# Two attention steps per turn of TensorE's loop, with another order of loads, casts and first steps

## The reference

```python
def _attn_ref(q, k, v, s):                       # (2, 8, 576, 64), s: (2, 8, 576)
    scores = scale * np.matmul(q, k.transpose(0, 1, 3, 2))
    s_pos = np.maximum(s, 0.0)
    cum = np.cumsum(s_pos, axis=-1)
    bias = -(cum[:, :, :, None] - cum[:, :, None, :])
    scores = np.where(causal, -1000000000.0, scores + np.minimum(bias, 0.0))
    attn = softmax of scores over the last axis
    return np.matmul(attn, v)

def reference(**kwargs):
    x = attention output, reshaped to (1152, 512)
    x = _moe_ref(x, ...)     # 8 experts, top 2 of noisy logits; relu(x @ w1[e]) @ w2[e]
    return _moe2_ref(x, ...) # 8 experts, dense, weights from 8 Sinkhorn steps
```

## Time and profile before

| | us |
|---|---|
| median of 3 runs | 1208.1 |
| lowest, highest | 1206.51, 1209.63 |
| profiled execution: its own time | 1210.0 |
| profiled execution: span of the core | 1208.3 |
| PE busy | 1191.1 (99%) |
| DVE busy | 696.7 (58%) |
| ACT busy | 421.9 (35%) |
| POOL busy | 259.8 (22%) |

### The profile page before, as it was taken

How to read it: one execution, slowest core, us unless ns; L and a number is a source line. 1 busy time by engine, 2 the same in 40 slices (tenths; PEclk the granted TensorE clock), 3 DMA queues, 4 the chain that set the end, 5 groups by cost and what they waited for, 6 DMA issues and landing times.

```text
span 1208.3 us, 20170 instructions
## 1 busy us (share of the span) xinstructions
PE 1191.1 (99%) x7149; PEld 1059.8 (88%) x7149; DVE 696.7 (58%) x1579; ACT 421.9 (35%) x887; POOL 259.8 (22%) x307
## 2 busy tenths in 40 slices
PE   8999899999999989999999999999999999999998
PEld 5888798888888888989889899899898898898997
DVE  5554676544544451566575575575575665755753
ACT  5666344433444341233133232242241231332320
POOL 8777111111101357111011011010010010110110
PEclk9999899999999999999999999999999999999999
DMA  7770644444545420012120210211211201202102
GB/s 171 164 186 21 246 136 156 153 153 180 179 171 201 160 79 1 1 36 79 62 70 0 69 55 15 69 35 35 69 35 35 69 14 56 69 0 69 35 0 78
DMA packets 40326, 103.04 MB, mean 85 GB/s; under 512 B 4814, under 2 KB 23758, under 8 KB 38106
## 3 DMA queue, kind: packets, MB, share of 16 engines
q1 hardware_dynamic: 33850, 85.97, 22.9%
q0 software_dynamic: 3360, 11.01, 3.1%
q10 hardware_dynamic: 3072, 5.51, 1.3%
HBM read 87.74 MB, written 10.30 MB: 81 GB/s over the span
## 4 chain that ended last, share of the span: by engine, by line
PE 94%; DVE 2%; POOL 1%; DMA 1%; ACT 1%; issue 0%; POOLq 0%; DVEq 0%
PE bank L1132 10%; PE bank L1131 10%; PE bank L1130 9%; PE bank L1086 9%; PE bank L1084 9%; PE bank L1085 9%; PE bank L909 5%; PE bank L911 5%; PE bank L910 5%; PE bank L891 5%; PE bank L893 4%; PE bank L892 4%; PE bank L820 4%; PE bank L803 1%; PE bank L769 1%; PE bank L804 1%
## 5 line engine op out<-in xcount | busy, mean ns | idle before, releaser
L740 POOL TENSOR_TENSOR part2l<-raw_part,part2h 128x512 fp32r<-128x512 f32 x56 | 72.5, 1294 | 589.7 <-ACT part2h L1365 589.7
L1132 PE MATMUL bank<-part2h,partl 128*128 128x512 f32 x504 | 198.6, 394 | 0.0
L1131 PE MATMUL bank<-part2l,parth 128*128 128x512 f32 x504 | 197.6, 392 | 0.0
L1130 PE MATMUL bank<-part2h,parth 128*128 128x512 f32 x504 | 195.6, 388 | 0.0
L1820 DVE SCALAR_TENSOR_TENSOR x_sb<-bank,share_now,x_sb 128x512 f32<-128x512 f32 x126 | 94.4, 750 | 159.4 <-PE bank L1132 159.4
L1086 PE MATMUL bank<-x_forms,forml 128*128 128x288 f32 x448 | 132.1, 295 | 0.0
L1084 PE MATMUL bank<-x_forms,formh 128*128 128x288 f32 x448 | 131.9, 294 | 0.0
L1085 PE MATMUL bank<-x_forms,formh 128*128 128x288 f32 x448 | 131.8, 294 | 0.0
L1505 DVE SCALAR_TENSOR_TENSOR hl<-bank,hh 128x336 fp32r<-128x336 f32 (+1 forms) x88 | 45.8, 521 | 131.4 <-ACT hh L1242 123.8
L891 PE MATMUL bank<-xTh,w1h 128*128 128x336 f32 (+1 forms) x352 | 115.8, 329 | 0.7 <-DVE xTl L1485 0.5
L892 PE MATMUL bank<-xTl,w1h 128*128 128x336 f32 (+1 forms) x352 | 113.8, 323 | 0.0
(11 more groups left out here) (229 smaller groups left out, 2455.3 us busy)
## 6 DMA issues: line engine op xcount, KB each, us to landing
raw<-in_w SPq DMA_DIRECT2D x15, 2048.0 KB, 9.2
raw_part<-in_w1b SPq DMA_DIRECT2D x14, 1024.0 KB, 6.0
raw_part<-in_w2b SPq DMA_DIRECT2D x14, 1024.0 KB, 6.1
k_raw<-in_kT SPq DMA_DIRECT2D x16, 288.0 KB, 5.3
y_dram<-x_sb ACTq DMA_DIRECT2D x16, 256.0 KB
q_raw<-in_qT SPq DMA_DIRECT2D x8, 288.0 KB, 5.1
q_two<-w2l SPq DMA_DIRECT2D x8, 288.0 KB, 6.0
x_dram<-x_sb SPq DMA_DIRECT2D x1, 2304.0 KB, 10.0
```

Source lines behind the costliest of these rows:

```text
L1130: pe.matmul(dst, parth[:, l, ts], part2h[:, l, :], start=(l == 0), stop=False)
L1131: pe.matmul(dst, parth[:, l, ts], part2l[:, l, :], start=False, stop=False)
L1132: mm = pe.matmul(dst, partl[:, l, ts], part2h[:, l, :], start=False, stop=(l == FL - 1))
```

## The change

The four jobs and what they compute stay as they are. What changes is order and place:

- **PE's loop** goes over pairs of steps from k = 0 on: both `rough`, both sets of turns, both `scores`, both `mix`, both token turns. The other engines keep their single steps.
- **The first steps** are laid out anew (`FILL` = 10, `roughs_at`, `turns_at`): the loop starts at k = -10, 7 instead of 10 `rough` stand before the first `scores`, and the distance of 13 steps is reached at k = 6. PE and DVE both follow `roughs_at`.
- **`HIGH_AHEAD`** goes from 19 to 21: ACT rounds k and q of heads 2 to 7 (and the first expert's w1) two steps earlier. The q of head 1 is rounded at k = -7 and -6.
- **Loads** of head 1 on are issued as k, k, q. `load_raw(1)` now stands behind the four `first_cum`, and `double_k(1)` behind the store of the sums, the load of v and `load_cum(1)`.
- **The running sums' low part** is computed before the rounding of k for the first head; that rounding (64x1152) moves from DVE to ACT.
- **Constant rows** of ring place 1 move from POOL to DVE (three memsets), and those of ring place 2 come earlier on POOL.
- `WARM_UPS` goes from 8 to 6 and `WARM_TOP2` from 18 to 15. Two semaphores are merged into one.

The numbers of the lines in the changed kernel are higher: `rough` L786, `turn_max` L800, `scores` L820 and L821, `mix` L837, `keep_warm` L843; on ACT `high_k` L1195, `high_q` L1204, `place_max` L1187, the exponentials L1176 to L1179.

The diff:

```diff
         MAX_BANKS, MAX_AT, SCORES_AT, OUT_AT = 3, 3, 4, 6
-        ROUGH_AHEAD, SCORES_AHEAD = 13, 4
-
-        WARM_UPS = 8
-        WARM_TOP2, WARM_RANKS, WARM_GATHER, WARM_BACK = 18, 4, 6, 29
+        ROUGH_AHEAD, SCORES_AHEAD, FILL = 13, 4, 10
+
+        WARM_UPS = 6
+        WARM_TOP2, WARM_RANKS, WARM_GATHER, WARM_BACK = 15, 4, 6, 29
...
-        HIGH_AHEAD, LOW_AHEAD = 19, 14
+        HIGH_AHEAD, LOW_AHEAD = 21, 14
...
         def high_at(k):
 
+            if k in (-7, -6):
+                return (1, 1, k + 7)
             h, part = divmod(k + HIGH_AHEAD, HEAD)
...
+        def roughs_at(k):
+
+            lags = {0: (10,), 1: (11, 12), 2: (13,), 3: (14, 15), 4: (16,), 5: (17, 18)}
+            r = lags[k] if k in lags else (k + FILL,) if k < 0 else (k + ROUGH_AHEAD,)
+            return [i for i in r if i < ALL]
+
         def turns_at(k):
 
+            early = {-7: (0, 0), -5: (0, 1), -2: (1, 0), 0: (1, 1)}
             first, rest = divmod(k + ROUGH_AHEAD - 4, STEPS), divmod(k + ROUGH_AHEAD - 7, STEPS)
-            found = []
-            if first[1] == 0 and 0 <= first[0] < G:
+            found = [early[k]] if k in early else []
+            if first[1] == 0 and 2 <= first[0] < G:
                 found.append((first[0], 0))
-            if rest[1] == 0 and 0 <= rest[0] < G:
+            if rest[1] == 0 and 2 <= rest[0] < G:
                 found.append((rest[0], 1))
...
             def load_raw(h):
                 w = h % RAW_RING
                 sp.dma_start(k_raw[0:HD, w, :], kT[h]).then_inc(k_loaded[w], 16)
-                sp.dma_start(q_raw[:, w, :], qT[h]).then_inc(q_loaded[w], 16)
+                if h == 0:
+                    sp.dma_start(q_raw[:, w, :], qT[h]).then_inc(q_loaded[w], 16)
                 sp.dma_start(k_raw[HD:P, w, :], kT[h]).then_inc(k_again[w], 16)
+                if h:
+                    sp.dma_start(q_raw[:, w, :], qT[h]).then_inc(q_loaded[w], 16)
...
             load_raw(0)
-            load_raw(1)
             sp.wait_ge(aug_ready, 2)
             sp.wait_ge(cum_high, 1)
             first_cum(HD, cum_h, 0, cum_first)
...
             first_cum(HD + 1, cum_l, 1, cum_loaded[0])
+            load_raw(1)
             double_q(0)
...
+            load_v(0)
+            load_cum(1)
             double_k(1)
-            load_cum(1)
-            load_v(0)
             sp.wait_ge(low, LOWS)
             load_raw(2)
...
+            for i, w in enumerate((0, 2)):
                 pool.memset(k_top[w][HD:P, :].bitcast(F32), 1.0).then_inc(aug_ready, 1)
                 pool.memset(q_top[w][HD:P, :].bitcast(F32), 0.0).then_inc(q_rows_clear, 1)
-                pool.wait_ge(q_rows_clear, w + 1)
-                pool.memset(q_top[w][HD:HD + 2, :].bitcast(F32), 1.0).then_inc(q_rows_ready, 1)
-
-            constant_rows(0)
-            constant_rows(1)
...
-            for k in range(-ROUGH_AHEAD, ALL):
...
-                if k + ROUGH_AHEAD < ALL:
-                    rough(k + ROUGH_AHEAD)
...
+            for ks in [(k,) for k in range(-FILL, 0)] + [(k, k + 1) for k in range(0, ALL, 2)]:
+                for k in ks:
+                    for r_ in roughs_at(k):
+                        rough(r_)
+                    if k < -SCORES_AHEAD:
+                        keep_warm(BANK // 2)
+                for k in ks:
+                    for n, part in turns_at(k):
+                        turn_max(n, part)
+                for k in ks:
+                    if 0 <= k + SCORES_AHEAD < ALL:
+                        scores(k + SCORES_AHEAD)
+                for k in ks:
+                    if k >= 0:
+                        mix(k)
+                for k in ks:
+                    if k >= EARLY_AT:
+                        if k == EARLY_AT:
+                            pe.wait_ge(head_done, G - 1)
+                        turn_token(SP_, k - EARLY_AT, x_sb)
...
             act.copy(cum_h[0:G, :], cum_s[0:G, :]).then_inc(cum_high, 1)
+            act.wait_ge(k_loaded[0], 16)
+            act.copy(k_top[0][0:HD, :], k_raw[0:HD, 0, :]).then_inc(k_first, 1)
+            for half in range(B):
+                high_q(0, half)
             for h in range(2):
                 for half in range(B):
-                    high_q(h, half)
-                for half in range(B):
                     high_k(h, half)
...
-            v.wait_ge(k_loaded[0], 16)
-            v.tensor_copy(k_top[0][0:HD, :], k_raw[0:HD, 0, :]).then_inc(k_first, 1)
             v.wait_ge(cum_high, 1)
             v.tensor_tensor(cum_l[0:G, :], cum_s[0:G, :], cum_h[0:G, :].bitcast(F32), ALU.subtract).then_inc(cum_low, 1)
+            v.memset(k_top[1][HD:P, :].bitcast(F32), 1.0).then_inc(k_rows_ready, 1)
+            link(v.memset(q_top[1][HD:P, :].bitcast(F32), 0.0))
+            v.memset(q_top[1][HD:HD + 2, :].bitcast(F32), 1.0).then_inc(q_second_ready, 1)
...
-                if k + ROUGH_AHEAD < ALL:
-                    row_max(k + ROUGH_AHEAD)
+                for r_ in roughs_at(k):
+                    row_max(r_)
```

More of the change, by code:

```diff
@@ L202, in build @@
         q_rows_ready = sem("q_rows_ready")
+        k_rows_ready = sem("k_rows_ready")
+        q_second_ready = sem("q_second_ready")
         k_again = [sem(f"k_again{w}") for w in range(RAW_RING)]
@@ L227, in build @@
         first_w1 = [sem(f"first_w1_{c}") for c in range(DC - 1)]
-        gates_loaded = sem("gates_loaded")
-        noise_loaded = sem("noise_loaded")
+        gates_noise_loaded = sem("gates_noise_loaded")
         dve = sem("dve")
@@ L439, in load_cum @@
                 w = h % HEADS_RING
-                if h < HEADS_RING:
-                    sp.wait_ge(aug_ready, 2 + h)
                 if h == 1:
+                    sp.wait_ge(k_rows_ready, 1)
                     sp.wait_ge(cum_stored, 32)
+                if h == 2:
+                    sp.wait_ge(aug_ready, 3)
                 sp.dma_start(k_top[w][HD:HD + 2, :].rearrange("r (b s) -> r b s", b=B).bitcast(F32),
@@ L587, in _, with q_ones @@
             pool.wait_ge(const_ready, 6)
-            def constant_rows(w):
+            def q_ones(w):
+                pool.memset(q_top[w][HD:HD + 2, :].bitcast(F32), 1.0).then_inc(q_rows_ready, 1)
+            for i, w in enumerate((0, 2)):
                 pool.memset(k_top[w][HD:P, :].bitcast(F32), 1.0).then_inc(aug_ready, 1)
                 pool.memset(q_top[w][HD:P, :].bitcast(F32), 0.0).then_inc(q_rows_clear, 1)
-                pool.wait_ge(q_rows_clear, w + 1)
-                pool.memset(q_top[w][HD:HD + 2, :].bitcast(F32), 1.0).then_inc(q_rows_ready, 1)
-            constant_rows(0)
-            constant_rows(1)
-            pool.wait_ge(aug_ready, HEADS_RING)
-            pool.wait_ge(q_rows_ready, 2)
+                pool.wait_ge(q_rows_clear, i + 1)
+                if w == 0:
+                    q_ones(0)
+            pool.wait_ge(aug_ready, 3)
+            pool.wait_ge(q_rows_ready, 1)
             def low_part(h, c, k):
@@ L641, in _ @@
                     pool.wait_ge(low, LOWS)
-                    constant_rows(2)
-                    pool.wait_ge(q_rows_ready, 3)
+                    q_ones(2)
+                    pool.wait_ge(q_rows_ready, 2)
                 if k >= 0:
@@ L754, in rough @@
                         pe.wait_ge(k_doubled[w], 16 * (h // HEADS_RING + (w > 0)))
-                    if h < HEADS_RING:
-                        pe.wait_ge(q_rows_ready, h + 1)
+                    if h == 1:
+                        pe.wait_ge(q_second_ready, 1)
+                    elif h < HEADS_RING:
+                        pe.wait_ge(q_rows_ready, 1 if h == 0 else 2)
                     if h == 0:
@@ L958, in _ @@
                 keep_warm(BANK)
-            for k in range(-ROUGH_AHEAD, ALL):
-                if k + ROUGH_AHEAD < ALL:
-                    rough(k + ROUGH_AHEAD)
-                if k < -SCORES_AHEAD:
-                    keep_warm(BANK // 2)
-                for n, part in turns_at(k):
-                    turn_max(n, part)
-                if 0 <= k + SCORES_AHEAD < ALL:
-                    scores(k + SCORES_AHEAD)
-                if k >= 0:
-                    mix(k)
-                if k >= EARLY_AT:
-                    if k == EARLY_AT:
-                        pe.wait_ge(head_done, G - 1)
-                    turn_token(SP_, k - EARLY_AT, x_sb)
+            for ks in [(k,) for k in range(-FILL, 0)] + [(k, k + 1) for k in range(0, ALL, 2)]:
[18 more added lines that the diff above has]
+                        turn_token(SP_, k - EARLY_AT, x_sb)
             pe.sem_inc(xg_turned, SLOTS_T)
@@ L1196, in _ @@
             act.copy(cum_h[0:G, :], cum_s[0:G, :]).then_inc(cum_high, 1)
+            act.wait_ge(k_loaded[0], 16)
+            act.copy(k_top[0][0:HD, :], k_raw[0:HD, 0, :]).then_inc(k_first, 1)
+            for half in range(B):
+                high_q(0, half)
             for h in range(2):
                 for half in range(B):
-                    high_q(h, half)
-                for half in range(B):
```

(6 more changed lines are left out.)

6 lines of the change are left out of this document (3 added, 3 removed).

## The result

The changed kernel is slower: 1252.6 us median of four runs (1246.49 to 1256.81) against 1207.6 before on the same chip, a ratio of 1.0365 with a 95% interval of 1.0342 to 1.0388. The forecast was 1209.4, the range 1204.5 to 1212.8. Where runs of one kernel lie far apart, a ratio counts only those near its fastest, so the runs are given beside it. The profiled execution took 1246.49.

The account below looks back on a forecast made before the run. PE was taken to bound the kernel, 94% of the span. Start +1.4, gate weights +1.25, end -0.55 and -0.3, pairs -0.5 made +1.3 us on 1208.1: forecast 1209.4, range 1204.5 to 1212.8.

Parts of the forecast that it names:

- rival (c): TensorE's clock falls after PE's idle time near 22 us, costing 1.7 to 3.4 us: 1211.1 to 1212.8; chance 0.14.
- The prediction's list of waits: PE's waits up to 145 us: few and short after 2.4 us, a single one between 30 and 118 us.
- The start, +1.4: Up to the turn (2,0): ACT held by loads, turn at 23.9 instead of 23.35; 1.4 us worse, bounds -1.8 and +4.
- The gate weights, +1.25: Split at step 60: PE waits 1.9 us at rough 76 instead of 0.66; +1.25 us, bounds 0 and 2.
- The end, -0.55 and -0.3: End of attention: last division starts earlier, -0.55 us; three products fewer before the ranks, -0.3 us.
- The pairs, -0.5: Steady state of the attention: paired steps save -0.5 us over seven heads, bounds -3.5 and +1.2.
- (a): Start: loads of heads 1 and 2 land sooner, ACT is not held, -1 instead of +1.4: 1207.0; chance 0.2.
- (b): Steady state: pairs are cheaper than counted, 0.1 us each: 1206.4; chance 0.08.
- (d): Start: DVE's memsets are held by POOL as the cast was, start +4: 1212.0; chance 0.08.

Follow-up runs that it names:

- e4_ahead19: Changed kernel with k doubled 19 steps ahead instead of 21, nothing else: 1249.8 to 1288.3 us in five runs, ratio 1.0382.
- e2_no_idle: Changed kernel with head 2's first k piece behind placement (1,1) and the gate-weight split spread over steps 61 to 67: 1241 to 1291 us.
- e3_cured: Changed kernel, gate split at step 53, one product of constants ahead of scores 0, two ahead of turn (2,0): ratio 1.0000.
- e4_mixed: Changed kernel, single steps up to 9, head 2's k from step 0, split at 53, one product of constants ahead of scores 0: ratio 1.0006.
- e1_fill_both: Changed kernel with two products of constants ahead of turn (2,0) and two ahead of rough 76: 1213.5, 1214.0, 1227.6, 1230.2 us.
- e3_old53: Kernel before in pairs with its own start, k doubled 21 steps ahead, gate split at step 53: ratio 0.9989.
- the pairs alone: Kernel before with only PE's order changed to pairs of steps from step 0 on: 1210.8, 1217.0, 1276.5, 1283.9 us.
- e2_pairs_old_start: Kernel before in pairs, own start, k doubled 21 steps ahead, split over steps 61 to 67: three of twelve over 1225 us, most others 1214 to 1224.
- e2_pause_dense: Kernel before with six ACT copies that pause PE near 23 us and five products of constants behind turn (2,0): 1216.7 to 1219.0 us.
- e4_dense: Changed kernel with the gate split at step 53 and five products of constants behind turn (2,0): 1214.5 to 1216.7 us.

## Why the prediction was wrong

**The step that failed is the price of the clock.** The sum of the forecast has no term for it, and rival (c), which has one, priced it far too low. Its mechanism, place and sign were right: PE idle before the turn (2,0), the clock under 1.00 between 17 and 35 us. I priced it by the one low stretch of before, 6.8 us, at 1.7 to 3.4 us, and gave it 0.14. The two low stretches of the changed kernel cost 30 to 31 us. In the row of before the low stretch lay in token turns and gate products; here it lies in the attention's own stream, in which the clock stayed low for 31, 38, 119 and, in `e4_ahead19`, 181 us. At 0.45 us each, that is 14 to 81 us for one fall, where the whole range was 8.3 us wide. The point from which it decides was wrong too: I said about 2 us of idle time, and `e2_no_idle` was low in six of six, in its profile with no wait over 1.13 us ahead of the fall. Nor does a count of PE's work sort the runs. It is 6.42 us in 20:30 of the changed kernel and 8.03 in `e2_no_idle`, for 9.17 in the kernel before, though part of the first two ran at half the clock, which lengthens them. But `e3_cured` had 7.90 at full clock and was undisturbed in ten of twelve runs, and `e4_mixed`, with 9.01, was low in six of twelve. So one wait of 1.91 us is shown to be enough, and what starts the falls without one stays open.

The prediction's list of waits also leaves one out, at the very place: in the kernel before a `mix` waits 0.83 us for POOL, up to 22.96.

```profile
PE bank L820 <- POOL probT L628: 0.8, 1, 0.8
```

**The start, +1.4.** The times of the steps came out near: first `rough` 9.80 (9.5 predicted), memsets 1.02 (1.1), the first row maximum 11.38 (10.5, since the small copy of `rinv` ahead of it took 0.81 us), the sums' copies landing in 1.7 to 1.9 us (2.8), ACT held to 13.84 (13.8), `scores` 0 at 17.32 (17.2), `rough` 10 at 20.37 (20.0), head 2's k 23.25 (22.6), the turn (2,0) at 24.54 (23.9). That makes +2.0 at this place. I did not follow it further: `rough` waits twice more for a row maximum (0.47 and 0.61 us in `e1_fill_both`, at full clock). Between `e3_cured` and `e3_old53`, which up to there differ mainly in the start and its fillers, the last token turns stand at 124.67 and 121.46: the new start costs 3.2, fillers included.

The Trainium skill's figure for the memsets, an estimated 1.2 us, lies above the 1.02 measured; the skill ("VectorE: DVE Perf Modes", the section on zero memsets) and the row differ by little and nothing hangs on it.

**The gate weights, +1.25.** The wait was 3.41 us, not 1.9: +2.75. The 1.9 is what the pairs alone showed (1.81). The rest goes with an edit that I had costed at nothing, `HIGH_AHEAD` 21: it moves ACT's rounding of w1 two steps ahead, with it POOL's `w1l`, and so beside the split. I had looked at ACT's room and not at what POOL then gets earlier. The clock fell at about the end of this wait, and with the split at 53, where the wait is gone, the profile has no such fall. With 38 us at 0.45 the wait was worth some 20 us in the end. How much of it the 1.9 us would have cost alone is open: the clock stayed up after 1.81 us in the pairs alone and fell in a wait of 1.93 us in `e2_pairs_old_start`.

**The end, -0.55 and -0.3.** The wait before the last token turns fell from 0.79 to 0.35 where the clock was full (0.2 predicted). The gain at the ranks did not come: PE waits 1.48 us for `chosen` in the changed kernel, 0.83 in `e3_cured`, and from the last token turns to there it is 17.13 us in `e3_cured` for 16.80 before.

**The pairs, -0.5.** Heads 3 to 7 are 12.67 us apart for 12.69, 0.1 in all. Where `e3_old53` reaches the last token turns, 1.64 us sooner than before, 0.66 is the split's and about 0.44 the end's; 0.5 is left for the pairs and the earlier k. Size and bounds were right, in a sum of small terms from single runs.

**(a), (b), (d)** are out: ACT was held twice; heads were no 0.4 us less apart; no memset was held.

At full clock the changed kernel would then be the start +2 to +3, the gates +2.75, the end and the pairs -0.6: some 1212 to 1213, and `e1_fill_both` had 1213.5, with four more products in it and a wait of 1.61 instead of 3.41. What lies above this is the clock.

## What to carry to other kernels

A wait on PE is priced twice: by its own length, and by the chance of a fall of the clock times how long the stream behind it keeps the clock low; the second is not read off a low stretch in other work. A step that can't be kept dense wants dense products right behind it, which cost about 1 us here. With them twelve runs of twelve were alike; without them it was ten of eleven, and beside them thirteen of nineteen of the kernel before. When a lead is changed on one engine, follow the data to every engine that then runs earlier, and look at what it will run beside.

## What the runs showed of the hardware

**Busy is not enough to bring the clock back.** From 30 to 50 us PE shows 9.5 to 10.0 of 10 us busy at 0.50. The Trainium skill ("TensorE: Matmul & The Clock Gate", Part 1) says that sustained matmul activity releases the clock to 2.4 GHz. By the profile's busy time that does not hold for this kernel's attention, for up to 181 us, while with five products of 512 columns behind the turn it was back about 3.4 us (`e2_pause_dense`) and 4 us (`e4_dense`) after the turn. Which property of the attention's stream keeps it low stays open: no run here changed the shape of its products.

**It is partly chance.** The same kernel ran 1207 and 1283 (`e3_old53`), and the kernel before was low in 20 of 90 runs. A median of three or four runs can fall on either side for a kernel near the edge.

**DVE can be held over many of POOL's operations.** `fold` took 0.16, 1.84 and 4.73 us, in step with POOL's unbroken run of `w1l` beside it. The Trainium skill ("SBUF — State Buffer", "SBUF: two separate sides") says that a DVE operation with two inputs in SBUF and a POOL operation that reads SBUF lock each other out, for the whole of an instruction. The rows agree in kind (`fold` reads `ident` twice, `w1l` is made from two tiles), but the 4.73 us last over ten of POOL's instructions, not one.
